# Ranks of the expert choice in PSUM, and masks of the next tile ahead of the index steps

## The reference

```python
for t in range(S):
    state = gamma[None, :, None, None] * state + np.einsum('bhd,bhe->bhde', k[:, :, t], v[:, :, t])
    y[:, :, t] = scale * np.einsum('bhd,bhde->bhe', q[:, :, t], state)
...
logits = x @ w_gate
expert_idx = np.argmax(logits, axis=1)
...
for i in range(N):
    e = expert_idx[i]
    if counts[e] < capacity:
        disp[e, counts[e]] = x[i]
        pos[i] = counts[e]
        counts[e] += 1
        keep[i] = True
h = np.maximum(np.einsum('ecd,edf->ecf', disp, w1), 0.0)
y = np.einsum('ecf,efd->ecd', h, w2)
...
g = P / (Q + 1e-06)
return (g @ w_out)
```

## Time and profile before

| | us |
|---|---|
| median of 3 runs | 536.71 |
| lowest and highest | 536.19, 537.21 |
| the profiled execution's own time | 536.48 |
| its span in the profile | 534.6 |
| busy in the span: PE, DVE, ACT, POOL | 525.8, 425.0, 329.2, 76.6 |
| attention stage (tiles 0 to 11) | about 0 to 78 |

### The profile page before, as it was taken

The page is one execution under the profiler, slowest core; times in us unless marked ns, Lnnn a source line. Parts: engine busy times, 40 slices in busy tenths (PEclk is TensorE's granted clock), DMA queues, the critical chain, the costliest instruction groups (busy, mean ns, idle before and its releaser), DMA issues.

```text
span 534.6 us, 8737 instructions
## 1 busy us (share of the span) xinstructions
PE 525.8 (98%) x3209; PEld 439.0 (82%) x3209; DVE 425.0 (79%) x759; ACT 329.2 (62%) x508; POOL 76.6 (14%) x74
## 2 busy tenths in 40 slices
PE   7999999999999999999999999999999999999997
PEld 5887888888888888888788888888888888888885
DVE  3678788695856759577989999998888888787886
ACT  2454546484655747557869867657566566655652
POOL 2433342360101101003010010004000000200000
PEclk9999999999999999999999999999999999999999
DMA  9999959959958494903060000003000000200002
GB/s 192 229 269 234 281 200 394 398 145 390 380 232 307 146 332 149 397 25 99 23 217 1 1 21 20 1 1 115 4 21 20 1 0 2 78 1 0 0 1 79
DMA packets 65055, 72.26 MB, mean 135 GB/s; under 512 B 41202, under 2 KB 41714, under 8 KB 65012
## 3 DMA queue, kind: packets, MB, share of 16 engines
q1 hardware_dynamic: 58596, 57.96, 34.7%
q0 software_dynamic: 3136, 9.46, 5.2%
q10 hardware_dynamic: 3280, 4.28, 2.3%
HBM read 59.09 MB, written 12.60 MB: 134 GB/s over the span
## 4 chain that ended last, share of the span: by engine, by line
PE 94%; DMA 2%; DVE 1%; issue 1%; SPq 1%; POOL 1%; ACT 0%; POOLq 0%
PE up_low L953 7%; PE up_low L954 7%; PE up_low L955 7%; PE bank L955 6%; PE bank L953 6%; PE bank L954 6%; PE up_high L959 5%; PE up_low L959 5%; PE yrows L953 4%; PE yrows L954 4%; PE up_high L955 4%; PE up_high L953 4%; PE up_high L954 4%; PE yrows L955 4%; PE up_low L960 2%; PE up_high L960 2%
## 5 line engine op out<-in xcount | busy, mean ns | idle before, releaser
L880 DVE TENSOR_TENSOR T<-raw,T 128x1024 fp32r<-128x1024 f32 x60 | 71.5, 1221 | 34.0 <-ACT T L874 34.0
L874 ACT ACTIVATE T<-raw 128x1024 fp32r<-128x1024 f32 x60 | 60.5, 1070 | 32.4 <-PE bank L955 32.0
L953 PE MATMUL up_low<-x2H,T 128*128 128x512 f32 x176 | 69.3, 394 | 0.0
L955 PE MATMUL up_low<-x2H,T 128*128 128x512 f32 x176 | 68.6, 390 | 0.0
L954 PE MATMUL up_low<-x2L,T 128*128 128x512 f32 x176 | 68.6, 390 | 0.0
L1533 ACT ACTIVATE sq<-up_low 128x512 f32<-128x512 f32 x44 | 26.2, 595 | 64.5 <-PE up_low L955 64.3
L1554 DVE SCALAR_TENSOR_TENSOR wa<-sq,coef,wa 128x512 f32<-128x512 f32 x48 | 36.0, 749 | 28.7 <-ACT wa L1535 28.7
L953 PE MATMUL bank<-T,hL 128*128 128x512 f32 x128 | 50.6, 395 | 0.0
L955 PE MATMUL bank<-T,hH 128*128 128x512 f32 x128 | 49.9, 390 | 0.0
L954 PE MATMUL bank<-T,hH 128*128 128x512 f32 x128 | 49.9, 390 | 0.0
L1547 ACT ACTIVATE rc<-wa,cst 128x512 f32<-128x512 f32 x48 | 34.8, 725 | 20.5 <-DVE wa L1554 15.7
(11 more groups left out here) (205 smaller groups left out, 1231.2 us busy)
## 6 DMA issues: line engine op xcount, KB each, us to landing
raw<-in_moe_w_dram SPq DMA_DIRECT2D x14, 2048.0 KB, 11.0
raw<-in_moe_w_dram SPq DMA_DIRECT2D x8, 512.0 KB, 5.1
w_out_raw<-in_moe_w_out_dram SPq DMA_DIRECT2D x4, 1024.0 KB, 17.0
ybuf<-ysb ACTq DMA_DIRECT2D x15, 256.0 KB, 5.6
qin<-in_q_dram SPq DMA_DIRECT2D x12, 256.0 KB, 5.0
kin<-in_k_dram SPq DMA_DIRECT2D x12, 256.0 KB, 5.8
vin<-in_v_dram SPq DMA_DIRECT2D x12, 256.0 KB, 5.5
xbuf<-xt SPq DMA_DIRECT2D x12, 256.0 KB, 4.1
```

The costliest lines, as they stand in the source:

```text
L874: e.activation(W[w][:, 0, cols], raws[par][:, w, cols], ACT.Copy).then_inc(r.wH[w], 1)
L880: e.tensor_tensor(W[w][:, 1, cols], raws[par][:, w, cols], W[w][:, 0, cols].bitcast(F32), ALU.subtract).then_inc(r.wL[w], 1)
L953: nc.tensor.matmul(out_, aL, bH, start=start, stop=False)
L955: return nc.tensor.matmul(out_, aH, bH, start=False, stop=stop)
```

## The change

The ranks are written to columns 24 to 31 of the tile's gate bank in PSUM, and rankv in SBUF is gone. mine is copied from hot_all, behind a wait for it, where it was computed from the ranks. In dve_tile the masks of the next tile (dve_mask) come ahead of dve_lane and dve_put.

```diff
-        rankv = sb(ctx, "rankv", [P, E])
...
             e.wait_ge(s_lg, t + 1)
-            logits = gate_bank(t)[:, 0:E]
+            logits, rankv = gate_bank(t)[:, 0:E], gate_bank(t)[:, 3 * E:4 * E]
             e.tensor_copy(lg_all[:, t, :], logits).then_inc(s_lc, 1)
             e.wait_ge(s_lc, t + 1)
             e.tensor_reduce(mx_all[:, t:t + 1], lg_all[:, t, :], AX.X, ALU.max).then_inc(s_pick, 1)
             e.wait_ge(s_pick, 3 * t + 1)
-            e.scalar_tensor_tensor(out=rankv[:, :], in0=logits, scalar=mx_all[:, t:t + 1], in1=cc("rank"),
+            e.scalar_tensor_tensor(out=rankv, in0=logits, scalar=mx_all[:, t:t + 1], in1=cc("rank"),
                                    op0=ALU.is_equal, op1=ALU.mult).then_inc(s_pick, 1)
             e.wait_ge(s_pick, 3 * t + 2)
-            e.tensor_reduce(rmax[:, :], rankv[:, :], AX.X, ALU.max).then_inc(s_pick, 1)
+            e.tensor_reduce(rmax[:, :], rankv, AX.X, ALU.max).then_inc(s_pick, 1)
             e.wait_ge(s_pick, 3 * t + 3)
-            e.tensor_scalar(hot_all[:, t, :], rankv[:, :], rmax[:, :], None, ALU.is_equal).then_inc(s_hot, 1)
+            e.tensor_scalar(hot_all[:, t, :], rankv, rmax[:, :], None, ALU.is_equal).then_inc(s_hot, 1)
             if t >= NT - LAST:
-                e.tensor_scalar(mine[t - (NT - LAST)][:, :], rankv[:, 0:1], rmax[:, :], None, ALU.is_equal).then_inc(s_fit, 1)
+                e.wait_ge(s_hot, t + 1)
+                e.tensor_copy(mine[t - (NT - LAST)][:, :], hot_all[:, t, 0:1]).then_inc(s_fit, 1)
...
                 dve_place(t - 1)
                 dve_count(t - 1)
+            dve_mask(t + 1)
+            if t >= 1:
                 dve_lane(t - 1)
                 dve_put(t - 1)
-            dve_mask(t + 1)
```

## The result

| | us |
|---|---|
| before, median of 20 runs | 536.23 (535.52 to 537.24) |
| changed, median of 20 runs | 537.77 (536.79 to 538.09) |
| ratio, 95% interval | 1.0026 (1.0020 to 1.0033) |
| the profiled execution of the changed kernel | 537.35, span 535.5 |

The change makes the kernel slower by 0.26%, or 1.5 us between the medians. That is more than the 0.2% that I had set as "no change", and 537.77 lies 0.07 us above my range. Microseconds in the text are differences of medians; whether a difference is clear of noise is read from the intervals.

What follows compares the result with a forecast made beforehand. PE bounds the kernel, busy 525.8 of 534.6 us, with lgT almost without slack. Terms -0.79 - 0.11 + 3 x 0.25 = -0.15 us on the profiled 536.48, with the runs' median 0.23 higher, gave 536.4 us, range 535.3 to 537.7.

Steps and rivals of the forecast that it cites:

- The price of PSUM: Reading the ranks from PSUM on DVE: costed at nothing, bound 0.1 us for the three instructions together.
- the third of the list in part two: Undisturbed tile, masks first: qs starts at 59.59, before tok, and holds it until 60.43.
- inside at 0.04 late: Undisturbed tile, masks first: vs on POOL holds inside until 59.43, 0.04 us lost.
- my 0.25 us a tile: Undisturbed tile, masks first: lgT comes at 60.58 instead of 60.33, so PE loses 0.25 us.
- the sign of the first rival: In the new profile, tok 0.24 us long throughout would mean that DVE gets through.
- the first rival: DVE keeps its turn against POOL's qs, so 0.75 us isn't paid: -0.90, 535.6 us; chance 0.25.
- three of the nine reordered: Count of reordered tiles with vs and qs spaced to lose 0.25 us each, together 0.75 us.
- The close tile: Tile with index steps at 35.28: tok first by 0.03 us, costed at nothing; if POOL is first, 0.9 later.
- the slow rival: POOL wins every meeting, inside held through vs and qs, close tile lost: +1.7 us, 538.2; chance 0.15.
- No DMA is moved: Claim that the change shifts no DMA; SP's next load of q may go out 0.05 us later.
- The gain of part one: Ranks in PSUM free hot_all from POOL's hold in the disturbed tile: 0.79 us, once.
- my sum had 0.90: Disturbed tile: gains of 0.79 us from hot_all unheld and 0.11 from the new order.

Runs made afterwards that it cites:

- the kernel before with its ranks moved: Kernel before, ranks still in SBUF but rankv allocated further up, so DMA buffers move down 32 bytes: 535.87 us beside 537.79, ratio 0.9962.
- the run with qs behind lane_hot: Changed kernel with one more wait, so that POOL starts qs only when lane_hot is done: 535.18 us beside 537.31, ratio 0.9962.
- before again: The kernel before, unchanged, run once more beside later experiments for its profile on their chip: 537.73 us beside 537.79, ratio 1.0002.
- qs behind tok: Changed kernel with one more wait, so that POOL starts qs only when tok is done: 535.31 us beside 537.31, ratio 0.9968.

## Why the prediction was wrong, point by point

**The reading of what bounds the stage held.** PE follows lgT without slack, some DVE instructions and POOL exclude each other, and the held one works from 0.2 us before POOL's end. The price of PSUM held as well: rmax is 167 ns against 161, hot_all 226 ns, and from the copy of the logits to hot_all it is 0.87 us (62.45 to 63.32) against 0.86 before. The rule of the Trainium skill ("VectorE: DVE Perf Modes", TRN2 errata) that spoke against the change, by my estimate 65 ns more per PSUM source, isn't seen here.

**The step that failed first** is the third of the list in part two: "qs starts at 59.59, before tok, and holds it". It is lane_hot that is held, the instruction in front of tok. I had put inside at 0.04 late and then jumped to tok; in fact inside is 0.12 late, lane_hot comes up at 60.48, and qs, straight behind vs at 60.49, has the turn. lane_hot is dispatched 0.20 before tok, and that is the difference between my 0.25 us a tile and the 0.44 measured in seven tiles. tok takes 0.23 or 0.24 in all twelve tiles. I had set that down as the sign of the first rival, DVE getting through, and DVE did not get through: the sign could not tell the two apart.

**The second** is the count: "three of the nine reordered". I counted tiles in which qs follows vs at once in a trace whose loads were slow and whose tiles were short. With tiles longer by 0.44 and loads faster, qs is there in time in eight of nine, every one that has a qs. The close tile of the earlier trace rows was lost with the others. Three tiles at 0.25 became seven at 0.44 and one at 0.86: 3.9 us instead of 0.75. So the slow rival was nearest in its direction, not in its mechanism: no tile had inside held by two POOL instructions in a row.

**The third** is a part that I didn't see at all. I took the removal of rankv for nothing, and it moved the DMA buffers: -1.9 us by the kernel before with its ranks moved. The prediction says "No DMA is moved", and that holds for the order of the issues alone. "DMA: Bandwidth & Descriptors" of the Trainium skill, section "How a descriptor splits into AXI transactions", could have warned me: a transaction has to start from a multiple of 256 bytes, and the first one of a descriptor that starts elsewhere begins at the boundary below, with bytes that are fetched and not used. The landings at 0, 32, 64 and 128 agree with it; the page has no price for a load like this one, and how the engine splits a transfer no run shows.

**The gain of part one** is the least certain term. hot_all is never held in the changed kernel, as forecast, but in its trace no POOL instruction runs while hot_all is due, so that trace doesn't test the mechanism. The one meeting that does is in the run with qs behind lane_hot (48.32, shown above), and there the mechanism holds. How often it pays depends on when loads land: before again shows one hold of tok and none of hot_all, where the first trace had one of each. Ranks in PSUM on top of moved buffers show no gain that the intervals can tell (0.9967 beside 0.9962). I had taken 0.79 us from a single execution as if it were there in each. Where the two first traces differ by that stretch (1.27 us, my sum had 0.90), it is because no qs came late after the change, and not because of PSUM.

**The sum** that the first two traces give goes by the starts of lgT. From the first to the tenth it is 52.71 us in the changed kernel (14.49 to 67.20), 50.04 before (15.81 to 65.85), and 48.77 with qs behind tok, where no hot_all, lane_hot or tok is held (14.71 to 63.48). So the held tiles cost 3.94 us, the disturbed stretch of before gives back 1.27, and the first lgT is 1.32 earlier. That makes +1.35, and the last lgT is 1.36 later (75.25 against 73.89). The medians differ by 1.5 (537.77 - 536.23). This sum was made after the result; it shows that the three parts account for the loss, and forecasts nothing.

## What to carry to other kernels

Before an instruction of DVE is moved, list what POOL does in the stretch that it moves into, instruction by instruction, and ask of each pair whether it can be held; count such meetings for the new pitch and not in the old trace. Ask also whether the meeting comes back: here DVE's lateness made PE late, and PE's made vs late, which kept the two side by side tile after tile. A buffer removed or added moves every buffer behind it: compare the addresses modulo 256 of whatever a DMA fills before a gain or loss is put down to the code. A stall that comes from a late load in one trace is a chance event, and its price has to be weighted by how often it comes.

## What the runs showed of the hardware that I had not expected

- Loads of 256 KB into SBUF landed in 4.4 to 5.1 us with buffers on multiples of 256 bytes, in 5.0 to 5.9 us at 32, 64 and 128 above, and going from 32 above to 0 was worth 0.38% of the kernel.
- POOL going from one instruction to the next kept its turn against a DVE instruction that came up 0.01 us before the second's recorded start (60.48 and 60.49), while inside, waiting since 60.22, was served between the two.
- In all twelve experiments, on three chips and with the kernel before among them, DVE stood idle for 1.4 to 1.5 us ahead of the second last lgT, and PE waited for it for about 1 us; in the first traces of before and after, from elsewhere, it was idle for 0.25 there. The row below is from the kernel before again. PE's product for it had ended 1.2 us earlier. No row says what DVE waited for; it is the same in all versions, and stays open.

```profile
72.41 0.29 DVE L503 COPY lgT<-up_high 128x128 f32<-128x128 f32 x1 [1.37 <-PE up_high L366]
```
